# A prologue of sixteen half heads of batch 0 in plain float32, in a one-core attention and MLP kernel

## The reference

```python
# 1 attention: window of 128 keys, a distance bias per head
scores = scale * np.matmul(q, k.transpose(0, 1, 3, 2))
bias = slopes[:, None, None] * (-np.abs(rel))[None, :, :]
mask = (rel >= 0) & (rel < window)
scores = np.where(mask, scores + bias[None], -1e9)
attn = softmax(scores); attn_out = np.matmul(attn, v)
# 2 first MLP (width 2048) on the layer-normalised x, with a residual
xn = (x - mu) / np.sqrt(var + 1e-06) * g_ln
x = x + np.maximum(xn @ w_ch1, 0.0) @ w_ch2
# 3 second MLP (width 1024): three-tap convolution along the sequence as a gate
h = np.maximum(x @ w_in, 0.0); gate = sigmoid(conv3(h))
out = (h * gate) @ w_out
```

## Time and profile before

| | |
|---|---|
| time, three runs | 837.19, 833.74, 836.97 us; median 836.97 |
| profiled execution | span of its instructions 834.8 us; 2.2 us under that median |
| PE busy / PE weight loads | 786.3 us (94%) / 765.4 us (92%) |
| DVE / ACT / POOL busy | 547.0 / 385.0 / 171.7 us |
| mean granted TensorE clock | 0.965 of full speed |
| DMA | 60.81 MB, mean 73 GB/s |

### The profile page before, as it was taken

The page is one execution under the profiler, slowest core; times in us unless marked ns, Lnnn a source line. Parts: engine busy times, 40 slices in busy tenths (PEclk is TensorE's granted clock), DMA queues, the critical chain, the costliest instruction groups (busy, mean ns, idle before and its releaser), DMA issues.

```text
span 834.8 us, 17035 instructions
## 1 busy us (share of the span) xinstructions
PE 786.3 (94%) x5792; PEld 765.4 (92%) x5792; DVE 547.0 (66%) x1510; ACT 385.0 (46%) x1063; POOL 171.7 (21%) x155
## 2 busy tenths in 40 slices
PE   4776788999999999999999999999999999999998
PEld 3665778999999999998999999999998999999998
DVE  4997677777367777645677754522229887788862
ACT  5775456565224655512556632122235444444442
POOL 4553675211011211101112200021120110111100
PEclk9676799999999999999999999999999999999999
DMA  5441554221122123013121201411312122221101
GB/s 154 106 130 48 156 162 127 60 78 43 58 65 66 38 71 101 8 58 102 29 71 51 86 8 61 134 58 54 89 49 76 31 79 78 78 78 47 59 22 44
DMA packets 64425, 60.81 MB, mean 73 GB/s; under 512 B 23904, under 2 KB 52576, under 8 KB 63840
## 3 DMA queue, kind: packets, MB, share of 16 engines
q1 hardware_dynamic: 64352, 59.87, 24.3%
HBM read 45.69 MB, written 14.16 MB: 72 GB/s over the span
## 4 chain that ended last, share of the span: by engine, by line
PE 69%; DVE 11%; issue 11%; POOL 3%; ACT 2%; DMA 2%; SPq 1%; POOLq 0%; DVEq 0%; ACTq 0%
PE bank L1009 20%; PE bank L1011 19%; PE bank L1010 19%; PE bank L950 4%; PE bank L964 3%; PE bank L980 3%; DVE prob L741 2%; DVE q_st L829 1%; DMA w_stage<-w 1%; DMA q_raw<-qT 1%; DVE ch_stage L741 1%; POOL rstd L482 1%; DVE rows L734 1%; ACT prob L562 1%; DVE rows L736 1%
## 5 line engine op out<-in xcount | busy, mean ns | idle before, releaser
L1009 PE MATMUL bank<-h_hi,wb_hi 128*128 128x288 f32 x512 | 156.9, 306 | 3.1 <-DVE h_lo L798 2.3
L1009 PE MATMUL bank<-xn_hi,wa_hi 128*128 128x288 f32 x512 | 157.0, 307 | 2.7 <-issue 1.4
L1010 PE MATMUL bank<-xn_lo,wa_hi 128*128 128x288 f32 x512 | 152.0, 297 | 0.0
L1011 PE MATMUL bank<-xn_hi,wa_lo 128*128 128x288 f32 x512 | 152.0, 297 | 0.0
L1011 PE MATMUL bank<-h_hi,wb_lo 128*128 128x288 f32 x512 | 151.6, 296 | 0.0
L1010 PE MATMUL bank<-h_lo,wb_hi 128*128 128x288 f32 x512 | 151.5, 296 | 0.0
L798 DVE SCALAR_TENSOR_TENSOR h_lo<-bank,h_hi 128x288 fp32r<-128x288 f32 x128 | 58.1, 454 | 109.8 <-ACT h_hi L594 108.5
L594 ACT ACTIVATE h_hi<-bank 128x288 fp32r<-128x288 f32 x128 | 52.3, 409 | 164.1 <-PE bank L1011 163.1
L1009 PEld LDWEIGHTS bank<-h_hi,wb_hi 128*128 128x128 f32 x512 | 97.1, 190 | 5.2 <-issue 3.9
L1009 PEld LDWEIGHTS bank<-xn_hi,wa_hi 128*128 128x128 f32 x512 | 97.6, 191 | 4.0 <-issue 3.2
L1010 PEld LDWEIGHTS bank<-xn_lo,wa_hi 128*128 128x128 f32 x512 | 97.7, 191 | 0.0
(11 more groups left out here) (95 smaller groups left out, 1752.0 us busy)
## 6 DMA issues: line engine op xcount, KB each, us to landing
k_raw<-kT SPq DMA_DIRECT2D x64, 144.0 KB, 2.8
q_raw<-qT SPq DMA_DIRECT2D x64, 144.0 KB, 2.9
w_stage<-w SPq DMA_DIRECT2D x32, 256.0 KB, 3.0
x_in<-x_spill SPq DMA_DIRECT2D x8, 580.0 KB, 4.3
ch_in<-ch_spill SPq DMA_DIRECT2D x8, 580.0 KB, 5.2
x_spill<-xT SPq DMA_DIRECT2D x4, 1152.0 KB, 5.3
ch_spill<-ch_stage SPq DMA_DIRECT2D x32, 144.0 KB, 1.9
out<-out_stage SPq DMA_DIRECT2D x32, 144.0 KB, 1.8
```

The source lines that it names most:

```text
L1009: nc.tensor.matmul(dst, w_h, a_h, start=start, stop=False)
L1010: nc.tensor.matmul(dst, w_h, a_l, start=False, stop=False)
L1011: last = nc.tensor.matmul(dst, w_l, a_h, start=False, stop=stop)
```

## The change

Only batch 0's attention, and what surrounds it, is changed; batches 1 to 3 compute as before.

- Batch 0 is cut into sixteen **half heads** (c, h): first the eight heads for queries 0 to 319 (c = 0, three tiles), then the eight for queries 320 to 575 (c = 1, two tiles). The norm of chunk 0 needs only the first eight. A half head's number is e = 8c + h.
- Its products are plain float32, with no hi and lo: HS (scores, 3 or 2 products), HP (5 or 4 float32 transposes into one bank), HO (3 products). The scores' operands have their lower 64 partitions zeroed and HO takes 128 columns of V, so most products are over 128 x 128.
- Before each HS, POOL scales q (`scale_q`, in the place of `k_lo` and `v_lo`). Row minima and the inverse of the sums stay on DVE; the multiplication by the inverse goes to ACT; P transposed is one DVE copy of 128x512 and the result one DVE copy into `xT`.
- **WARM**: products of the zeroed `h_hi`, 128x512, type fp32r, into bank 7, which nothing reads: 9 at the start, 8 ahead of the first HP, then 2 in each slot.
- `timeline("prologue")` is now slots of 1.0, one half head in each, and stops at slot 14.9. HO of e = 13, HP and HO of e = 14 and 15, as far as they lie behind that, and the norm of chunk 1 are in `first`. The heads of batch 1 begin at 8.5 in place of 6.5. The prologue has seven banks in turn.
- q and k come interleaved (`qkT`), one DMA per half head; four buffers of q, k and v. `w1` and `w_in` are laid out in DRAM tile by tile, so that a row of a tile is 2 KB in one piece (before: four pieces of 512 B).
- SP issues the first K, Q, V of batch 1 and the spill of x of batch 0 within `first`; the zeroing of the paddings of `pt_hi` and `pt_lo` moves behind the last HS.

```diff
-FRAME_PROLOGUE = {("S", "A"): 0.0, ("S", "B"): 0.5, ("S", "C"): 1.0, ("O", "A"): 1.5, ("O", "B"): 2.0, ("PT", "A"): 2.51, ("PT", "B"): 4.0}
+HALF_PROLOGUE = {("HS", 0): -0.3, ("HS", 1): -0.28, ("HP", 0): 1.8, ("HO", 0): 2.75}
+PROLOGUE_END = 14.9
+HALF_FIRST = [(-1.2, ("HP", 1, 6, 0)), (-0.3, ("HO", 1, 5, 0)), (0.4, ("HP", 1, 7, 0)), (0.6, ("HO", 1, 6, 0)), (1.6, ("HO", 1, 7, 0))]
+FIRST_NORM_PROLOGUE, FIRST_NORM_0 = 10.6, 2.4
+FIRST_HEAD_0, HEAD_SLOTS_0, LAST_NORM_0 = 8.5, 5.05, 56.2
+WARM_START = 9
+WARM = [(1.79, 8)] + [(m + 0.78, 2) for m in range(2, 15)]
...
-FIRST_W, W_SLOTS, W_PACE = 5.3, 6.0, 0.8
+FIRST_W, W_SLOTS, W_PACE = 0.9, 1.5, 0.8
...
+            def half_normalise(c, h):
+                e, r = half_no(c, h), half_rows(c, h)
+                act.wait_ge(half_sum, 2 * e + 2)
+                for t in range(HNT[c]):
...
+                    nc.scalar.activation(probs, probs, ACT.Copy, scale=row_inv[0:rows, r + t:r + t + 1]).then_inc(half_prob, 1)
...
+            def half_pt_copy(c, h):
...
+                nc.vector.tensor_copy(half_pt[e % 2][:], bank[bank_of(0, ("HP", c, h, 0))][:]).then_inc(half_pt_ready, 1)
...
+            def warm(n, dst):
+
+                for _ in range(n):
+                    nc.tensor.matmul(dst[:], h_hi[:, 0, 0:P], h_hi[:].rearrange("p s c -> p (s c)")[:, 0:512], start=True, stop=True)
...
+                for t, at in HGROUPS[c][x]:
+                    rows, q0, k0, keys, _, _ = HTILES[c][t]
+                    last = nc.tensor.matmul(dst[0:rows, at:at + keys], half_qk[e % 4][:, 0, q0:q0 + rows],
+                                            half_qk[e % 4][:, 1, k0:k0 + keys], start=True, stop=True)
...
+                for i, (j, n, src, cols, col) in enumerate(HPARTS[c]):
+
+                    m = D if j == 2 else 2 * D
+                    last = nc.tensor.matmul(dst[0:m, col:col + cols], half_v[e % 4][0:n].rearrange("p j d -> p (j d)")[:, D * j:D * j + m],
+                                            half_pt[e % 2][0:n, src:src + cols], start=i == 0, stop=i == 2, skip_group_check=True)
```

More of the change, by code:

```diff
@@ L95, in head_items, with half_items @@
     return out
+def half_items(c, start, slots, at, heads):
+    return [(start + slots * h + t, (kind, c, h, x)) for h in heads for (kind, x), t in at.items()
+            if kind != "HS" or x < len(HGROUPS[c])]
 def norm_items(start, c, times=NORM_TIMES):
@@ new lines, in take_bank @@
+            def take_bank(batch, item):
+                if is_int(batch) and (batch, item) in EARLY_NO:
+                    at = EARLY_NO[batch, item]
+                    same = [i for i in range(at) if EARLY_BANK[i] == EARLY_BANK[at]]
+                    if same:
+                        released(*EARLY_USES[same[-1]])
+                    return
+                late = [(0, x) for x in HEAD_ORDER] + [(0, (k, c, j)) for c in range(2) for k, j in NORM_ORDER]
+                at = late.index((0, item)) - 2
+                released(batch if at >= 0 else batch - 1, late[at][1])
@@ new lines, in half_prob_t @@
+            def half_prob_t(c, h):
+                take_bank(0, ("HP", c, h, 0))
+                dst = bank[bank_of(0, ("HP", c, h, 0))]
+                if c == 0 and h == 0:
+                    pe.wait_ge(identity_ready, 2)
+                    pe.wait_ge(zeros_ready, 4)
+                pe.wait_ge(half_prob, tile_of_half(c, h, HNT[c] - 1) + 1)
+                for t, k0, col in HBLOCKS[c]:
+                    rows, _, _, _, _, pcol = HTILES[c][t]
+                    last = nc.tensor.transpose(dst[:, col:col + rows], half_prob_of(c, h)[0:rows, pcol + k0:pcol + k0 + P],
+                                               ident[0:rows, 0:rows])
+                last.then_inc(bank_filled, 1)
@@ L1015, in first_product @@
                 c, f = divmod(k, F1)
-                if is_first(batch) and c == 0 and half == 0:
+                if is_int(batch) and batch == 0 and c == 0 and half == 0:
                     wait_w_split(pe, 2 * f)
@@ L1021, in first_product @@
                     pe.wait_ge(h_ready, STEPS * batch + k - 1)
+                if is_int(batch) and batch == 0 and k < 2 and half == 0:
+                    after_prologue(2 + k)
                 last = product(hid_bank[k % 2][:, 0:CH],
@@ L1036, in second_product @@
                     pe.wait_ge(ch_dve, 1 + 2 * (2 * batch + c))
+                if is_int(batch) and batch == 0 and k == 0:
+                    for d in (2 * half, 2 * half + 1):
+                        after_prologue(4 + d)
                 for d in (2 * half, 2 * half + 1):
```

525 lines of the change are left out of this document (369 added, 156 removed).

## The result

The changed kernel took 822.33 us (median of four runs, 820.9 to 822.66) against 837.08 for the kernel before beside it: ratio 0.9833, interval 0.9811 to 0.9855. It is faster by 1.7%, in the direction forecast; but of the 32 us forecast less than half came (14.75), and 822.3 lies above the range's end of 820.

A forecast was written before the change was run, and what follows sets the result against it. DVE first limits the prologue, PE at half clock close behind; PE's work bounds the rest. 834.8 - 29.0 + 3.0 - 2.9 - 3.0 = 802.9 us span, plus 2.2 gives 805; range 797 to 820.

The forecast's parts named there:

- part 2: Prologue slot, c=0: PE work 2.67 us at the higher clock, slot taken as 3.2 us, eight slots 25.6 us.
- part 3: Prologue, c=1 with norm: 18.0 us from HP 8 to HP 13, first MLP product at 60 us.
- part 5: Start of the MLP part: higher clock -2.9 us, half of the idle time taken back -3 us.
- part 4: Work moved behind first MLP product: HO of e = 13, 14, 15 and HP of e = 15, +3.0 us.
- rival B: Prologue slots of c=1: the clock falls, +14 us, time 819, or 822 with slow MLP start; chance 0.19.
- rival D: Prologue: PE never leaves the lower clock, 5.6 us per c=0 slot, first product at 91.5, time 843.5; chance 0.06.
- one chain: Prologue slot's dependent steps, HP e, DVE copy, inverse, multiplication, hand-overs, until HP e + 1: 3.0 us; 2.9 before HP 14.
- inverse 0.4: Prologue slot: DVE's inverse of the row sums, 0.4 us in the chain and in DVE's sum.
- The clock: Start of the MLP part: if PE arrives at the higher clock, 6 us at 0.52 become faster, -2.9 us.
- The stalls: MLP part, 100 to 140 us: half of PE's 6.4 us idle taken back, -3 us; bounds -6.4 and +6.4.
- rival C: MLP part stalls longer, 9.7 us more than taken, time 815; chance 0.06.

The follow-up runs named there:

- experiment 1: Changed kernel without the two products of zeros in each slot (those at the start and before the first transposes stay): 816.51 us, ratio 0.9774.
- experiment 4: Changed kernel with all HS and HO products over the full array (result not the reference's): 817.86 us, ratio 0.9789.
- experiment 3: Changed kernel with four products of zeros in each prologue slot in place of two: 823.52 us, ratio 0.9849.
- experiment 5: Changed kernel without DVE's addition of 1e-9 to the row sums in the half heads: 814.14 us, ratio 0.9731.
- experiment 12: Changed kernel without slot zeros or 1e-9 additions, larger HS/HO shapes, HO 13 ahead of HP 14, paddings later, GpSimd's inverse and DVE's apply ahead: 805.50 us.
- experiment 6: Changed kernel with POOL's writes of zeros to the paddings moved later, behind the first weight gains: 821.92 us, ratio 0.9819.
- experiment 10: Changed kernel with w1 in its layout of before, pieces of 512 bytes: 820.21 us, ratio 0.9813.
- experiment 9: Changed kernel with GpSimd's inverse root of blocks 1 and 2 ahead of `v_lo`, DVE's apply ahead of weight tile 18: 822.41 us, ratio 0.9811.
- experiment 7: Changed kernel with q and k of batches 1 to 3 in separate layouts again: 820.34 us, ratio 0.9805.

## Why the prediction was wrong

Three steps of it failed: PE's sum for a slot (part 2, 3.5 of the 18.0 us), the small step of DVE taken for granted (parts 2 and 3, 2.8 us), and the 5.9 us that part 5 took back in the MLP part as if they were certain (chunk 0 came 7.3 us over the forecast, 1.2 of it by part 4). The first two are shown by experiments; of the third it is known what didn't come, and only in part why. The sections behind chunk 0, where nothing was forecast, add 4.6 us, and that stays open.

**What was right.** The first transposes came at 12.74 (12.5 predicted). Float32 makes four passes (0.87 us for 512 columns). In the slots PE fills the time and the clock stays at 1.00 from the first one on; rivals B and D, the clock falling in the slots, didn't happen, and by experiment 1 it wouldn't have without zeros either. HP 14 came one chain behind HP 13 (3.1 against 2.9). No HS or HO of the slots waited for a DMA. The prediction's 3 to 8 tenths for PE in the first slices is 4 to 7 in its row, and it is the first slice's clock of 9 tenths that it passes over; nothing hangs on either.

The Trainium skill (TensorE: Matmul & The Clock Gate, Part 4: PE-mode transpose) says that transposes don't count as busy in the same way for the clock gate, which was the rule beside rival B. By this rule slots would have been lost; in none of these runs was one, zeros or not, though transposes are 0.7 of the 3.3 us of a slot without zeros. Float32 products stood between the transposes in every slot, so the rule itself isn't refuted.

**Part 2, the step that failed: PE's 2.67 us in a slot of c = 0, and the 3.2 taken from it.** The slot was 3.78, and all of it PE's. I counted columns streamed and cycles per column and left out what lies between products. The 1.11 us that were missing in the slot shown are, measured:
- 0.81 for products smaller than their neighbours: 0.56 in HS and HO (experiment 4: 1.32 + 1.21 down to 1.08 + 0.90), and 0.25 in the transposes, which took 0.68 with two small ones among five and the forecast 0.43 at c = 1, with four full ones;
- 0.17 for what HS and HO take beyond their columns in full shape (1.08 for 0.96, 0.90 for 0.85);
- 0.14 for the zeros, 0.57 in place of 0.43. I had put the slot on the chain's limit (3.0 to 3.2), beside which they cost nothing. With PE as the limit each pair cost its length, 0.50 and 0.47 us (experiments 1 and 3: 3.28, 3.78, 4.25 us).

Eight slots took 29.9 us in place of 25.6: 4.3 us. Only the first five are of this kind; the other three have the shorter HS of c = 1 in them, which I had not reckoned. And 0.8 of the 4.3 is not PE's but the addition's of 1e-9, since without it the same eight took 29.1 (experiment 5). Without zeros, and with one output product and two transposes still small, a slot takes 2.93 us (experiment 12), 0.7 more than the 2.24 of my figures without zeros: what lies between the products is about a quarter of such short work. Whether PE alone holds it there isn't shown, for ACT was busy for all of the 4 us from 20 to 24.

The Trainium skill (TensorE: Matmul & The Clock Gate, Step-by-step: what each phase is for) has PE pull weight loads ahead of running products, where the row groups don't conflict or the load goes to the background buffer. For neighbours of one shape the trace agrees (no idle ahead of a load in experiment 4's HS and HO). The loads of the 64-wide products came after 0.23 to 0.33 us of idling; whether one of these two conditions failed there, and what the cause inside PE is, no run here shows.

**Part 3, the second step that failed: 18.0 us from HP 8 to HP 13.** It was 20.0. The first four of these slots took 15.1 us together, the 15.1 of the forecast; the excess is in the last, 4.9 us in place of 2.9, with DVE's addition of 2.23 us in it. Without additions the five slots took 17.8 us (experiment 5), so the rest of this part was right. I took "inverse 0.4" for granted from one row at 12 us, where POOL was idle. That the addition is held up is shown by experiment 5 (without it HP 13 comes 3.0 us earlier), and that it waits for POOL's steps by experiment 6 (the writes of zeros moved away, it ended with `wb_lo`). The trace of before had the hint already, in the same step for a whole head:

```profile
27.81 0.61 DVE L734 TENSOR_SCALAR rows<-rows 128x2 f32<-128x2 f32 x1
```

This ended 0.02 us behind a step of POOL (27.36 to 28.40), as did two more of 0.62 us at 44.76 and 61.70, where the others took 0.14 to 0.17. The page's groups give only means, and I never asked for the range of L734. Behind HP 14 (3.1 us) I had 1.0 us to the first MLP product; it took 0.38.

The Trainium skill (SBUF — State Buffer, Who interferes with whom) has VectorE and GpSimd contend for a shared pair of ports that one instruction holds whole, and counts `tensor_scalar` among the operations that can take it. The trace agrees in the main, with 0.98, 1.05 and 1.20 us for tiny additions that ended 0.02 us behind POOL's `wb_lo`. The 2.23 us, over three steps of POOL, are more than one instruction. And of six additions that began beside POOL's scaling of q, on 64 partitions, only one (0.43 us) lasted to its end; the others took 0.16 to 0.37.

**Part 4: +3.0.** HO 13, 14, 15 and HP 15 took 1.7 (at the lower clock), 1.1, 1.1 and 0.35 us from start to start: 4.25. The same mis-sizing as in part 2, and the clock.

**Part 5, the third step that failed and the dearest: −2.9 and −3.** Chunk 0 was to be 2.9 us shorter with part 4 and is 4.4 longer: 1.6 us more of busy PE than reckoned, and 5.7 more of idle PE.

The clock: I had written "if PE arrives at the higher clock" and counted it as certain. It arrived after 3.1 idle of 4 us, and ran at a mean of 0.72 for 6 us, in place of 0.52: by an estimate from these two, 1.2 of the 2.9 us came. Experiment 12, with 1.1 idle of the 5 us from 52 to 57, shows the term was real (1.00 in that place).

The stalls: I took back half for two reasons, and neither held. The 2 KB pieces change nothing (experiment 10), and PE idles 9.3 us in chunk 0, before 6.6. The wait at 92 us alone is 3.5: the apply of blocks 1 and 2 stands behind GpSimd's root and a weight tile. But experiment 9 shows that removing it gives 0.9 us in the chunk and nothing in the time: the next waits lie right behind. In the stretch at 100 to 110 DVE has 9.0 and POOL 9.3 of 10 us; that was so before too. Which step there sets the time is not shown.

So rival C, the MLP part with longer stalls, is the one that came. I had priced it at 9.7 us more of stalls than I took, and PE idled 8.2 more over the whole MLP part; I gave it 0.06, and it came together with a longer prologue, which no case of mine had.

**What stays open.** The looped batches took 282.0 us against 278.9, with an unchanged program. Their PE idles 6.0 us in place of 3.5, in waits of DVE of 0.5 to 0.8 us each. Over the experiments it was 279.0 to 282.7, by the same code, and experiments 1, 7 and 12 exclude the layout. One execution of before was profiled, so how far its 278.9 wanders isn't known either. That DVE and POOL meet in another phase is my guess; I have no run that shows it. Nor is it shown why chunk 0's clock falls in one kernel and holds in another behind waits of like places.

## What to carry to other kernels

When PE is to become the limit, its sum has to be made from start-to-start times of sequences, not from columns over the clock: for products of 64 to 256 columns the rest was a quarter, and a product smaller than its neighbours cost a quarter of a microsecond more than a full one. Products of zeros that keep the clock up are free only where PE idles; check first that the stretch loses its clock without them. A tiny VectorE step on a chain of dependent work may take as long as GpSimd's step beside it, and a mean over its group hides that, so ask for its longest time; take it off the chain or use an operation that isn't held up; and a wait taken out in a stretch where the other engines are 90% busy is not a gain until the next one is named.

## What I had not expected of the hardware

- Three products are faster when the smallest of them is made as large as the others: HS 1.08 against 1.32 us, HO 0.90 against 1.21. In HO the load's 64 columns made 0.23 of the difference and its 64 rows 0.08 (experiment 12).
- A VectorE addition on 128x2 or 128x3 elements took 0.15 to 0.20 us alone and 0.98 to 2.23 beside GpSimd's `wb_lo`, up to the end of a GpSimd step, while RECIPROCAL of the same tile took 0.14 to 0.21 us.
- Without products of zeros the clock stayed at 1.00 from 12 to 57 us (experiment 1), with PE busy 93% of the time, 83% from 48 us on, and 0.7 us of each slot's 3.3 in transposes.
- A prologue 4.15 us longer cost the kernel 1.2 us (experiment 3), since the section behind it was 2.8 us shorter, at a mean clock of 0.96 in place of 0.94.
